# Small logit copy moved from ScalarE to VectorE, and other batches at the end, in a three-stage kernel

## The reference

```python
for t in range(S):                      # q, k, v, a_re, a_im: (4, 8, 768, 48)
    ar, ai = a_re_n[:, :, t, :, None], a_im_n[:, :, t, :, None]
    new_re = ar * S_re - ai * S_im
    new_im = ar * S_im + ai * S_re
    S_re, S_im = new_re + einsum('bhd,bhe->bhde', k[:, :, t], v[:, :, t]), new_im
    y[:, :, t] = einsum('bhd,bhde->bhe', q[:, :, t], S_re)
# x = y as 3072 tokens of 384; then tokens with x @ w_skip > 0 go through one of 8 experts
e_idx = argmax(xc @ w_gate, axis=1)     # gate_w: softmax of the logits at e_idx
out[do_compute] = xc + gate_w * (relu(xc @ w1[e]) @ w2[e])    # 384 -> 1024 -> 384
# last: every token through a feed-forward block 384 -> 2048 -> 384
h = x @ w_in;  result = (h * sigmoid(h)) @ w_out
```

## Time and profile before

| | us |
|---|---|
| median of 3 executions | 863.42 |
| all executions | 863.38, 863.42, 867.81 |
| the profiled execution | 867.81 |
| its span, first to last instruction | 866.1 |
| TensorE matmul busy in it | 821.0 (95%) |
| TensorE weight loads busy | 733.6 (85%) |
| VectorE busy | 360.3 (42%) |
| ScalarE busy | 343.5 (40%) |

### The profile page before, as it was taken

The page is one execution under the profiler, slowest core; times in us unless marked ns, Lnnn a source line. Parts: engine busy times, 40 slices in busy tenths (PEclk is TensorE's granted clock), DMA queues, the critical chain, the costliest instruction groups (busy, mean ns, idle before and its releaser), DMA issues.

```text
span 866.1 us, 12999 instructions
## 1 busy us (share of the span) xinstructions
PE 821.0 (95%) x5086; PEld 733.6 (85%) x5086; DVE 360.3 (42%) x674; ACT 343.5 (40%) x636; POOL 159.0 (18%) x196
## 2 busy tenths in 40 slices
PE   1399999999998899999999999999999999999997
PEld 0278888888897689999998999999999999999997
DVE  1588888889785212234213132132132132132112
ACT  6888988897642021111112222222222222222221
POOL 3111122623404155455000001001001001001001
PEclk9899999999998699999999999999999999999999
DMA  9999799576532768999530000001001001001001
GB/s 170 153 194 255 84 138 127 105 103 84 170 133 85 197 168 224 231 269 227 150 71 1 1 1 36 1 1 37 1 1 38 0 1 37 1 1 37 1 0 37
DMA packets 174998, 77.32 MB, mean 89 GB/s; under 512 B 152424, under 2 KB 168136, under 8 KB 174928
## 3 DMA queue, kind: packets, MB, share of 16 engines
q1 hardware_dynamic: 170000, 60.55, 35.4%
q0 software_dynamic: 4928, 15.84, 6.2%
HBM read 60.81 MB, written 15.59 MB: 88 GB/s over the span
## 4 chain that ended last, share of the span: by engine, by line
PE 89%; DVE 3%; issue 2%; ACT 2%; DMA 2%; POOL 1%; another core or an unknown queue 0%; DVEq 0%; SPq 0%; POOLq 0%; ACTq 0%
PE f_pU L1706 23%; PE f_pO L1712 23%; PE e_pH L1442 9%; PE e_pY L1456 8%; PE sc L549 5%; PE kvp L563 3%; PE yp L581 3%; PE yp L583 2%; PE sc L599 2%; PE tq L531 2%; PE tk L536 2%; PE cs L506 2%; PE cs L519 1%; PE cs L520 1%; DMA ring<-in_a_im 1%
## 5 line engine op out<-in xcount | busy, mean ns | idle before, releaser
L1706 PE MATMUL f_pU<-f_xT,wi 128*128 128x512 f32 x864 | 215.1, 396 | 0.8 <-DVE f_xT L1647 0.8
L1712 PE MATMUL f_pO<-wo,gT 128*128 128x384 f32 x1152 | 213.8, 336 | 0.0
L1712 PEld LDWEIGHTS f_pO<-wo,gT 128*128 128x128 f32 x1152 | 202.6, 188 | 7.5
L1706 PEld LDWEIGHTS f_pU<-f_xT,wi 128*128 128x128 f32 x864 | 161.5, 188 | 32.3 <-DVE f_xT L1647 1.2
L1663 DVE TENSOR_TENSOR gT<-g,gT 128x512 fp32r<-128x512 f32 x96 | 66.5, 692 | 286.5 <-ACT gT L1690 279.4
L1685 ACT ACTIVATE g<-f_pU 128x512 f32<-128x512 f32 x96 | 57.4, 598 | 298.2 <-PE f_pU L1706 298.2
L1653 POOL DMA_INDIRECT out<-o,row_of x24 | 24.1, 1004 | 428.7 <-DVE o L1674 422.3
L1442 PE MATMUL e_pH<-e_xT,ring 128*128 128x224 f32 x384 | 76.3, 360 | 0.0
L1442 PEld LDWEIGHTS e_pH<-e_xT,ring 128*128 128x128 f32 x384 | 74.5, 195 | 0.4
L1456 PE MATMUL e_pY<-hT,ring 128*128 128x224 f32 x384 | 74.1, 353 | 0.0
L1456 PEld LDWEIGHTS e_pY<-hT,ring 128*128 128x128 f32 x384 | 72.1, 190 | 0.0
(11 more groups left out here) (180 smaller groups left out, 967.2 us busy)
## 6 DMA issues: line engine op xcount, KB each, us to landing
ring<-in_moe_w SPq DMA_DIRECT2D x16, 1536.0 KB, 9.9
ring<-in_a_re SPq DMA_DIRECT2D x8, 576.0 KB, 8.7
ring<-in_a_im SPq DMA_DIRECT2D x8, 576.0 KB, 8.5
ring<-in_q SPq DMA_DIRECT2D x8, 576.0 KB, 8.1
ring<-in_k SPq DMA_DIRECT2D x8, 576.0 KB, 8.5
vraw<-in_v SPq DMA_DIRECT2D x8, 576.0 KB, 6.3
xs<-zero SPq DMA_DIRECT2D x9, 343.9 KB, 8.7
part<-in_moe_w_in POOLq DMA_DIRECT2D x12, 256.0 KB, 6.4
```

Source lines behind the costliest of these rows:

```text
L1706: mm = pe.matmul(pU[f % 2][:, :], wi[:, pw, c, f * 128:(f + 1) * 128], xT[b % 2][:, px, c, :], start=(k == 1), stop=(k == NK * len(TERMS)))
L1712: mm = pe.matmul(pO[t][:, 0:DM], gT[f % GB][:, pg, t * 128:(t + 1) * 128], wo[:, pw, f, :], start=(f == 0 and k == 0), stop=(f == NF - 1 a ...
```

## The change

The copy `lg_out` is taken out of ScalarE's list and becomes a `tensor_copy` on VectorE. There `lg_out(n - 2)` stands first in step `n`, ahead of `state(n)`, so one step later than ScalarE had it. It waits for `x_out(n - 2)`, so that its count still covers both reads of the bank. The last two copies come after the loop, and for chunk 47 alone the order of the two reads is turned round: `lg_out` waits for `turn_back` and `x_out` for `lg_out`. TensorE's waits are as before. The batches at the end become tiles 18 to 20, tile 21, and tiles 22 and 23 (they were 18 to 21, 22, and 23).

```diff
--- before.py
+++ after.py
@@ -21,7 +21,7 @@
         self.DM = X.shape[2] - EXTRA
         self.NK = self.DM // 128
         self.U = 6
-        self.batches = [(0, 6), (6, 6), (12, 6), (18, 4), (22, 1), (23, 1)]
+        self.batches = [(0, 6), (6, 6), (12, 6), (18, 3), (21, 1), (22, 2)]
         self.RANKS_AT = 256
         self.PAD = self.NT * 128
         self.ZEROS = self.R * REGION
@@ -742,18 +742,13 @@
                 if n < 0:
                     return
                 g, c = n // NC, n % NC
-                act.wait_ge(s["back_turned"], n + 1)
+                if n < LAST - 1:
+                    act.wait_ge(s["back_turned"], n + 1)
+                else:
+                    act.wait_ge(s["lg_out"], n + 1)
                 y = back[n % 2][:, 0:PAIRS * TW].rearrange("p (i e) -> p i e", i=PAIRS)[:, :, 0:D2]
                 x = X[:, (g // 2) * NC + c, (g % 2) * HD:(g % 2 + 1) * HD].rearrange("p (i e) -> p i e", i=PAIRS)
                 act.activation(x, y, ACT.Copy).then_inc(s["x_out"], 1)
-
-            def lg_out(n):
-
-                if n < 0:
-                    return
-                act.wait_ge(s["back_turned"], n + 1)
-                act.activation(parts(n), back[n % 2][:, 0:PAIRS * TW].rearrange("p (i e) -> p i e", i=PAIRS)[:, :, D2:TW],
-                               ACT.Copy).then_inc(s["lg_out"], 1)
 
             def before(p, c):
                 if c == 0:
@@ -806,10 +801,8 @@
                     before(p, c)
                     q_out(n + 2)
                     x_out(n - 1)
-                    lg_out(n - 1)
                     after(p, c)
             y_out(LAST - 1)
-            lg_out(LAST - 1)
             x_out(LAST - 1)
 
         def vector(dve):
@@ -902,6 +895,17 @@
                 dve.wait_ge(s["y_done"], n)
                 dve.tensor_tensor(U[(c + 1) % 2][0:D2, :, :], UK[0:D2, :, :], decay, ALU.mult)\
                     .then_inc(s["u_done"], 1)
+
+            def lg_out(n):
+
+                if n < 0:
+                    return
+                if n < LAST - 1:
+                    dve.wait_ge(s["x_out"], n + 1)
+                else:
+                    dve.wait_ge(s["back_turned"], n + 1)
+                dve.tensor_copy(parts(n), back[n % 2][:, 0:PAIRS * TW].rearrange("p (i e) -> p i e", i=PAIRS)[:, :, D2:TW])\
+                    .then_inc(s["lg_out"], 1)
 
             def choose(b):
                 t, u = routing.batches[b]
@@ -997,12 +1001,15 @@
             for p in periods():
                 for c in range(NC):
                     n = p * NC + c
+                    lg_out(n - 2)
                     state(n)
                     first(p, c)
                     s_out(n + 1)
                     between(p, c)
                     k_out(n + 2)
                     last(p, c)
+            lg_out(LAST - 2)
+            lg_out(LAST - 1)
             choose(5)
             routing.mark(dve, s, 5, link)
             routing.run(dve, s, 5)
```

## The result

The changed kernel takes 886.2 us (median, 884.4 to 889.3), the kernel before beside it 864.3: 1.025 times, 95% interval 1.0207 to 1.0291. The forecast was 878.4 with a range to 885.0. TensorE waits for the moved copy as predicted, in 37 places. But the waits are 3 us longer than forecast, and two losses that the sum had at nothing came on top: a lower clock after some of the gaps, and a late start of the experts' stage. The profiled execution took 890.25 us against 867.81, 22.4 more.

The account below looks back on a forecast made before the run. The prediction took the first stage to be bound by TensorE, which would wait for the late copy: 14.0 us in 38 waits plus 0.95 at the stage's end, 15.0 on the median 863.42, gives 878.4 us, range 871.5 to 885.

Parts of the forecast that it names:

- All of what follows hangs on the last scatter: After the first stage: experts and feed-forward have the same work, so nothing was added beyond the last scatter's delay.
- the 15.0 of the sum: Whole kernel: 14.0 us of waits for the copy plus 0.95 at the end of the first stage.
- What bounds the kernel, and what is removed: First stage: bound by TensorE; taking 48 copies of 0.181 us off ScalarE is worth nothing.
- What a copy costs: Moved copy on VectorE: 0.16 us plus 0.04 for the signal, so TensorE goes on 0.20 us after VectorE is free.
- A closed turn: Steps 3 and 4, VectorE and TensorE waiting for each other: 4.23 us where TensorE needs 4.09, 0.14 lost each.
- The Trainium skill's figure: Moved copy from PSUM on VectorE: 0.144 us by the page's formula, against the 0.16 taken.
- The steps of a period: First stage, scores waiting for the copy: 1.20 us a period, 2.19 with choose, 2.82 in period 6; 14.0 in 38 waits.
- step 0 of period 7: First step after period 6: scores wait for the copy, signalled at 256.08 but wanted at 254.58, 1.50 us.
- Rival 2: TensorE's clock also falls after gaps at 250 and 256 us: +4 to +8, some 884 us; chance 0.15.
- The end of the stage: Last batches: -0.32 us as the ranks' wait goes, +1.27 for the last batch's second scatter; together +0.95.
- The unknown piece of 4.30 us: At 264.74 us in the profiled chain, cause unknown; likely missing from other executions, so the sum was added to the median.
- Rivals 1 and 3: 1: only large delays count, 873.0 us, chance 0.15; 3: VectorE early enough, not slower, 864.4 us, chance 0.08.

Follow-up runs that it names:

- e16: Changed kernel plus unread matmuls in TensorE's five longest gaps and 48 one-element writes ahead of VectorE's first work: 880.5 us.
- e17: Kernel before with the new batches, copy left on ScalarE, and 96 one-element writes ahead of VectorE's first work: 863.9 us, 0.9962 of the kernel before.
- e1: Kernel before with only the new batches at the end, copy left on ScalarE: 863.2 us, 0.9946 of the kernel before.
- e8: Kernel before with the new batches, and loads of idle rows issued only once VectorE has begun the experts: 865.7 us, 0.9999 of the kernel before.
- e14: Kernel before with the new batches and 48 one-element writes ahead of VectorE's first work: 866.9 us, 1.001 of the kernel before.
- e3: Changed kernel with each of the 48 copies on VectorE made one step sooner: 872.6 us, 1.0059 of the kernel before.
- e12: Changed kernel with the copies on VectorE one step sooner, and ahead of choose and the fourth guard in those steps: 869.1 us.

## Why the prediction was wrong in size

Two steps failed beside a term that was too small. "All of what follows hangs on the last scatter" put the start of the experts' stage at nothing, and the clock stood in a rival in place of the sum. In the profiled executions the waits were 3.0 us more than forecast, the clock lost 3.0, and the start 2.2. The waits alone would have left the time in the range: with the clock and the start mended (e16) the kernel takes 880.5 us, 16.6 more than e17, against the 15.0 of the sum.

- **What bounds the kernel, and what is removed: right.** ScalarE's relief brought nothing that can be seen: e16 is above e17 by what its waits hold.
- **What a copy costs: too small.** The copy was 0.167 us, 0.16 by the slope between two copies. But the signal was set at 0.04 us, from one place where TensorE stood idle for 10 us ahead of transposes. Here it is 0.11 to the load, so 0.28 us in all and not 0.20. A closed turn loses 0.21 and not 0.14. One reading of a signal, ahead of another kind of instruction, carried a term that stood 38 times. That the kind of instruction or the idle time makes the difference isn't shown.
- **The Trainium skill's figure.** For the copy (VectorE: DVE Perf Modes, "The TRN2 errata") it gave 0.144 us; this trace has 0.167, and the measurement decides. On the signal, its page Perfetto Trace Analysis ("Summary: the profiler window per engine type") says that the propagation of a semaphore lies outside the time shown for an instruction; the 0.11 us between the end of the copy and the load agree in kind, and that page has no figure.
- **The steps of a period: right in kind.** Predicted and measured waits, us: period 0 1.20, 2.05; 1 1.20, 1.49; 2 2.46, 3.04; 3 1.20, 1.17; 4 2.46, 3.05; 5 1.20, 1.17; 6 2.82, 3.47; step 0 of period 7 1.50, 1.59. The sum was 14.0 in 38 waits, and is 17.03 in 37. 0.07 in each is 2.7. The other 0.3 is what is left of larger errors with both signs. Period 0, for which I took period 4's list, loses 1.39 us in step 2, as VectorE has another 1152 columns there (1.36 us from 59.17), and nothing in step 1. Step 4 of period 6 loses 0.61 and not 0.14: two guards (0.25 and 0.31 us) stand ahead of the products, which I overlooked. The choose steps lose 1.45 and not 1.17. Periods 3 and 5 come out as predicted only because two errors cancel: their turns lose more, and their step 2 loses 0.31, not 0.59. Where a step 0 after mark has lost 0.34 us already, steps 1 and 2 lose only 0.52 more, together 0.86; without such a step 0 they lose 0.79 to 0.84 in periods 1, 2, 4 and 6. It looks like the same lateness of VectorE, which my sum counted twice.
- **Rival 2 was not another case but a part of this one.** I gave the clock 0.15 as an alternative. It came beside the waits: 1.3 to 1.6 us each time at 63 us, and about 1.6 more in some executions. The gap of 1.39 us in period 0, which I had at 0.6, set off the first; it follows 0.5 us of idle time at 59 us, so that TensorE was busy 4.2 of the 6 us from 58 to 64. The gaps that I had named for it, at 250 and 256 us, are the ones that set it off in some executions only.
- **The end of the stage: half right.** The last scatter starts 1.28 us behind the other, as said. The -0.32 did not come: the ranks still waited 0.38 us. From chunk 46 to the last scatter it is -0.23, not +0.95. The kernel before had 0.87 us of a stall at scores 47 there, which the changed kernel's here and eight more of the 18 profiled executions lack. With the new batches and the copy on ScalarE the same distance is 1.47 us longer than before in e1, 0.08 shorter in e8 and 1.3 shorter in e14 and e17, so one trace can't price this term.
- **"All of what follows hangs on the last scatter": failed.** VectorE began late for a reason that hangs on the place of its code, 2.2 us later than in the profiled execution before, and 5 to 6 us later than in an early start. I had not counted the 48 new instructions as a shift of all later code.
- **The unknown piece of 4.30 us** was taken as absent in the median. What nine profiled executions lack is 0.87 us at that place. What the rest of the scatter of the kernel before is (863.3 to 870.4 over all runs) stays open: early and late starts have that size, but e1 (867.4) and e17 (867.2) were as slow in an execution with an early start.
- **Rivals 1 and 3 failed.** The small delays of 0.2 us count in full. VectorE was early enough only at both ends (up to scores 2, and from scores 44 on) and in the steps 0 with no mark before them.

From my own profiled forecast: 882.8 + 3.0 (waits) + 3.0 (clock) + 1.0 (start-up) - 1.2 (end) + 2.2 (start) - 0.6 = 890.2, and 890.25 was measured.

## What to carry to other kernels

A copy that moves to another engine is priced by when it is done in each step, and by the signal of the very pair of engines that waits: e3 and e12 did the same work for a quarter and a twentieth of the loss. Gaps of over a microsecond on TensorE are to be priced with the clock that may follow them, not as a case of their own: here the one in period 0 cost 1.3 to 1.6 us more in every profiled execution without filling, the two at the end of period 6 together about 1.6 us in some, and the two at choose nothing. And where a program jumps over code, a change of a few dozen instructions anywhere ahead moves the code behind the jump, which was worth 3 to 6 us here; a time that differs by so much from the waits in the trace should be looked for there.

## What the runs showed of the hardware

- The start of an engine behind a jump depends on the place of its code: 6.8 to 7.6 us after the last scatter with the jump at 499 (five profiled executions), 10.6 to 15.2 at 451 with the loads in place (seven). The Trainium skill (Runtime: NRT & Kernel Launch, "Instruction fetch mechanics") says that a taken branch to a target outside the fetched window forces a fetch before execution goes on. These runs agree in kind: the start was late with the jump at one place, and came with its data when the code stood elsewhere or the block was gone. The late starts were 3.3 to 7.0 us behind their data. That the time is a fetch is inferred, as the profile names no wait there. I had not weighed that page.
- Whether other DMA slows such a start stays open: without eight loads in that stretch it came at 9.89 us, once, against 10.63 to 15.15 with them.
- A second copy right behind a first one cost 0.08 us in the loop (4.38 against 4.30), not its 0.17.
- From the end of VectorE's copy to TensorE's weight load 0.11 us passed, where the earlier trace rows showed 0.04 from a product to transposes.
